# Moving the running sum of two of four experts from VectorE to GpSimd

## The chip, the core and the metric

The kernel runs on one core of a Trainium2 chip. The metric is the device time of one execution in microseconds (us). Three executions of the kernel before took 1468.2, 1460.78 and 1466.7 us; their median is 1466.7 us. Five engines work side by side, each through its own list of instructions in order: PE (TensorE, matmuls), DVE (VectorE), ACT (ScalarE), POOL (GpSimd) and SP (SyncE, which only issues DMAs here). They wait for one another through semaphores.

## What is computed

The reference has three stages; the first works step by step through a sequence of 768 tokens for 4 x 8 heads, the second is a soft mixture of four experts over 3072 tokens, the third sends each token to one of eight experts.

```python
# stage 1, per head
y[t] = q[t] @ state
state = state + beta[t] * outer(k_n[t], v[t] - state.T @ k_n[t])
# stage 2, x of 3072 x 384, four experts, F = 1024
p = domain_probs / (domain_probs.sum(-1, keepdims=True) + 1e-09)
for e in range(4):
    h = np.maximum(x @ w1[e], 0.0)
    out += p[:, e:e + 1] * (h @ w2[e])
# stage 3: token n goes to the expert with the largest logit
out[mask] = gate_w[mask, None] * (np.maximum(x[mask] @ w1[e], 0.0) @ w2[e])
```

The change is in `out += p * (h @ w2)` of stage 2: the sum over the four experts.

## The kernel before

Stage 2 goes through six tiles of 512 tokens, t = 0 to 5. Within a tile, each expert's 1024 hidden columns are cut into eight blocks, so a tile has 4 x 8 = 32 steps s (SPT) and the whole stage 192 steps n (NSTEP). In a step PE does `up(n)` (nine matmuls of 128x512, L1161 to L1163) and then `down(n - 1)` (nine more, L1174 to L1176). Precision is kept by splitting each operand into a high and a low part: ACT makes the high part of the step's weights (`w_high`, L532, tile wsh), and the low part wsl = raw - wsh is made by POOL (`low`, L426) or by DVE (`w_low`, L773). `up(n)` waits for the low part of its own weights, two steps after it was asked for: the loops call `low(n + 2)`. The hidden activations are split the same way by ACT (L536, hh) and DVE (`h_low`, L768, hl).

Stage 1 runs inside stage 2: during tile t the sequence chunk t + 1 is solved, and for chunk t + 2 a 32x32 triangular system is inverted. That inversion (`invert`, L247 and L250) is a chain of 62 dependent instructions of 128x31 up to 128x256 elements. For chunks 2 to 5 it stands on POOL, begun at step 18 + LATE[t] of tiles 0 to 3, with LATE = 3, 1, 0, 0. For the ten steps from there, `low_by_vector` gives the low parts of the weights to DVE, and POOL takes them again afterwards. In tiles 4 and 5 there is no inversion. The order on every engine is written out by the loop over n in `gpsimd`, `vector`, `scalar` and `tensor`; nothing rearranges it.

At the end of an expert, `drain(t, e)` on DVE takes the three PSUM banks ps_yt (128x512 each), multiplies them by the expert's probabilities pb into `acc` (e = 0) or `tmp` (e = 1, 2, 3), L798, and for e = 1, 2, 3 adds tmp to acc, three instructions of 128x512, L805. It stands at the steps s = 8, 16 and 24, and for e = 3 at s = 0 of the next tile. Semaphore dr_ok counts the multiplications; PE waits for it before it overwrites a bank. x2_ok counts the last expert's additions, and sum_ok those of e = 1 and 2.

Of the kernel before, what the change touches and what calls it, by code (L numbers as in the profile page):

```python
# [9 lines left out]
ALU = mybir.AluOpType  # L10
# [14 lines left out]
def f32(ap):  # L25
    return ap.bitcast(F32)


def program(nc, keep, kq_d, kn_d, vn_d, beta_d, probs_d, w_soft, w_top, emb, tau, out, p_d, xs, table):

    NC, _, D, _, _ = kq_d.shape
    E1, NF, _, WCOLS = w_soft.shape
    E2 = w_top.shape[0]
    N, DM = out.shape
    KM = DM // P
# [23 lines left out]
    def sb(stack, name, shape, dt=F32):  # L59
        return stack.enter_context(nc.sbuf_tensor(name, shape, dt))  # L60

    def sem(name):
        return keep.enter_context(nc.semaphore(name))
# [25 lines left out]
    with ExitStack() as soft:  # L89
# [4 lines left out]
        acc = sb(soft, "acc", [P, 2, KM, TOK])  # L94
        tmp = sb(soft, "tmp", [P, KM, TOK])
# [83 lines left out]
    psum_ok, rp_ok, p_set = sem("psum_ok"), sem("rp_ok"), sem("p_set")  # L179
    wh_ok, wlp_ok, wld_ok = sem("wh_ok"), sem("wlp_ok"), sem("wld_ok")  # L180
    s1, hi_ok, lo_ok, s2, y_mm = sem("s1"), sem("hi_ok"), sem("lo_ok"), sem("s2"), sem("y_mm")
    dr_ok, sum_ok, x2_ok = sem("dr_ok"), sem("sum_ok"), sem("x2_ok")
    whT_ok, wlT_ok = sem("whT_ok"), sem("wlT_ok")

    r_const, r_iota, r_dve, r_en, r_enr, r_ent, r_entc = (sem("r_" + n) for n in
# [23 lines left out]
    def att_slot(t, s):  # L209
        return s - LATE[t]  # L210
# [5 lines left out]
    def low_by_vector(n):  # L216
        return n >= 2 and inverting(n - 2)
# [160 lines left out]
    def gpsimd(pool):  # L378
        def constants():
            iota = dict(allow_small_or_imprecise_dtypes=True)  # L380
            nc.gpsimd.memset(upper[:, :], 1.0).then_inc(ones_set, 1)
            nc.gpsimd.memset(upper2[:, :], 1.0).then_inc(ones_set, 1)
            nc.gpsimd.memset(upper3[:, :], 1.0).then_inc(ones_set, 1)
            nc.gpsimd.memset(identR[:, :], 0.0).then_inc(ones_set, 1)
            nc.gpsimd.memset(TT[:, :, :], 0.0).then_inc(zero_set, 1)
            pool.wait_ge(ones_set, 4)
            for mask, base in ((upper, BLK), (upper2, -BLK), (upper3, HALF + BLK)):
                nc.gpsimd.affine_select(out=mask[:, :], in_=mask[:, :], compare_op=ALU.is_gt, fill=0.0, base=base,
                                        pattern=[[1, HALF]], channel_multiplier=-1).then_inc(half_set, 1)
            pool.wait_ge(half_set, 3)  # L390
            nc.gpsimd.affine_select(out=identR[:, :], in_=identR[:, :], compare_op=ALU.not_equal, fill=1.0, base=0,
                                    pattern=[[-1, P]], channel_multiplier=1).then_inc(mask_set, 1)
            pool.wait_ge(mask_set, 1)
            nc.gpsimd.tensor_copy(upper[0:BLK, :], upper2[0:BLK, :]).then_inc(mask_set, 1)
            pool.wait_ge(mask_set, 2)
            nc.gpsimd.tensor_copy(upper[P - BLK:P, :], upper3[P - BLK:P, :]).then_inc(mask_set, 1)
            pool.wait_ge(mask_set, 3)
            nc.gpsimd.memset(ones[:, :], 1.0).then_inc(r_iota, 1)
            nc.gpsimd.memset(after[:, :], 1.0).then_inc(r_iota, 1)
            nc.gpsimd.memset(fill[:, :, :].rearrange("p r c -> p (r c)"), 0.0).then_inc(r_iota, 1)  # L400
            pool.wait_ge(r_iota, 3)
            nc.gpsimd.affine_select(out=after[:, :], in_=after[:, :], compare_op=ALU.is_gt, fill=0.0, base=0,
                                    pattern=[[1, P]], channel_multiplier=-1).then_inc(r_const, 1)
            nc.gpsimd.memset(fill[:, :, 0:1], float(N)).then_inc(r_const, 1)
            nc.gpsimd.memset(zrow[:, :], 0.0).then_inc(r_const, 1)
            nc.gpsimd.iota(rev[:, :], [[-1, E2]], base=E2, channel_multiplier=0, **iota).then_inc(r_const, 1)
            nc.gpsimd.iota(eoff[:, :], [[N, E2]], base=0, channel_multiplier=0, **iota).then_inc(r_const, 1)
            nc.gpsimd.iota(run[:, :], [[N, E2]], base=0, channel_multiplier=0, **iota).then_inc(r_const, 1)
            nc.gpsimd.iota(ids[:, :], [[P, NT], [ROWS, SUB]], base=0, channel_multiplier=1, **iota).then_inc(r_const, 1)
            nc.gpsimd.memset(starts[:, :], 0).then_inc(r_const, 1)  # L410
            nc.gpsimd.memset(oh[:, SUB, :], 0.0).then_inc(r_const, 1)

        def values(c):
            pool.wait_ge(brn_ok, c + 1)
            pool.wait_ge(v_in, 16 * (c + 1))
            nc.gpsimd.tensor_tensor(vN[:, :, :], vN[:, :, :], brn[:, c % 2, :].unsqueeze(2).to_broadcast([P, NU, D]),
                                    ALU.mult).then_inc(v_ok, 1)

        def mask_scores():
            pool.wait_ge(pc_ok, VN)  # L420
            nc.gpsimd.tensor_tensor(PT[:, :, :], PT[:, :, :], upper[:, :].unsqueeze(1).to_broadcast([P, NU, HALF]),
                                    ALU.mult).then_inc(p_ok, VN)

        def low(n):
            pool.wait_ge(wh_ok, n + 1)
            nc.gpsimd.tensor_tensor(wsl[:, n % WB, :], raw[:, n % RB, :], f32(wsh[:, n % WB, :]),  # L426
                                    ALU.subtract).then_inc(wlp_ok, 1)

        def scatter(t):
            pool.wait_ge(r_slot, t + 1)  # L430
            for j in range(SUB):
                nc.gpsimd.indirect_dma_start(  # L432
                    out=table[:, :],
                    out_offset=bass.IndirectOffsetOnAxis(ap=slot_i[:, t % 2, j:j + 1], axis=0),
                    in_=payload[:, t % 2, j, :], in_offset=None).then_inc(scattered[t % 2], 16)

        constants()
        values(0)
        mask_scores()
        for n in range(2):  # L440
            low(n)
        invert(pool, nc.gpsimd, 1)
        values(1)
        for n in range(NSTEP):
            t, s = divmod(n, SPT)
            a = att_slot(t, s)
            if n + 2 < NSTEP and not low_by_vector(n + 2):
                low(n + 2)
            if t >= 1 and s == ROUTE + 9:
                if t == 1:  # L450
                    pool.wait_ge(fill_out, 16)
                scatter(t - 1)
            if a == INV_SLOT and t + 2 < NC:
                values(t + 2)
                invert(pool, nc.gpsimd, t + 2)
        scatter(NT - 1)
        top_gpsimd(pool)

# [187 lines left out]
    def vector(dve):  # L646
# [133 lines left out]
        def drain(t, e):  # L780
            i = E1 * t + e
            dve.wait_ge(pb_in[i % 2], 16 * (i // 2 + 1))
            if e == 0 and t >= 2:
                dve.wait_ge(r_lg, SUB * (t - 1))
            if i == 1:
                dve.wait_ge(fill_out, 16)
                dve.wait_ge(xs_zero, 16)
            if e == 1 and t:
                dve.wait_ge(x2_ok, KM * t)
            if e > 1:  # L790
                dve.wait_ge(sum_ok, KM * ((E1 - 2) * t + e - 1))
            for kk in range(KM):
                if kk < KM - 1:
                    dve.wait_ge(y_mm, (KM - 1) * i + kk + 1)
                else:
                    dve.wait_ge(s2, NF * (i + 1))
                dst = acc[:, t % 2, kk, :] if e == 0 else tmp[:, kk, :]
                nc.vector.tensor_tensor(dst, ps_yt[kk][:, :], pb[:, i % 2, :], ALU.mult).then_inc(dr_ok, 1)  # L798
            for kk in range(KM):
                if e:  # L800
                    dve.wait_ge(dr_ok, KM * i + kk + 1)
                if e > 1:
                    dve.wait_ge(sum_ok, KM * ((E1 - 2) * t + e - 2) + kk + 1)
                if e:
                    nc.vector.tensor_tensor(acc[:, t % 2, kk, :], acc[:, t % 2, kk, :], tmp[:, kk, :],  # L805
                                            ALU.add).then_inc(x2_ok if e == E1 - 1 else sum_ok, 1)

        def probabilities():
            dve.wait_ge(p_in, 16)
# [115 lines left out]
        for n in range(NSTEP):  # L925
            t, s = divmod(n, SPT)
# [569 lines left out]
    @block.gpsimd  # L1496
    def _(pool):
        gpsimd(pool)
# [14 lines left out]
def build(nc, kq, kn, vn, beta, probs, w_soft, w_top, emb, tau, out):  # L1513
    N, DM = out.shape
    xs = nc.dram_tensor("xs_scratch", (N + P, DM), F32, kind="Internal").ap()
    table = nc.dram_tensor("slot_table", (w_top.shape[0] * N, 2), F32, kind="Internal").ap()
    p_d = nc.dram_tensor("p_scratch", tuple(probs.shape), F32, kind="Internal").ap()
    with ExitStack() as keep:  # L1518
        program(nc, keep, kq, kn, vn, beta, probs, w_soft, w_top, emb, tau, out, p_d, xs, table)
# [47 lines left out]
```

## Time and profile before

| | value |
|---|---|
| median of three executions | 1466.7 us |
| profiled execution, its own time | 1468.2 us |
| its span on the core | 1466.4 us |
| PE busy | 1333.3 us, 91% |
| DVE busy | 658.5 us, 45% |
| POOL busy | 592.5 us, 40% |
| ACT busy | 471.2 us, 32% |
| mean granted clock of PE, of full speed | 0.954 |

A row of a group of instructions reads: line, engine, operation, output <- inputs, shapes and count; then busy time and mean duration in ns; then the idle time of that engine just before these instructions, and which engine's instruction ended it. A row in order of time begins with the start in us from the start of the span and the duration in us; neighbours of the same kind are merged (x3), and the idle time ahead of it stands in brackets. A matmul row's duration overlaps the next row's, so PE's speed is read from the distance between starts.

### The profile page before, as it was taken

What the parts mean: (1) busy time and instruction counts of PE and PEld (TensorE: products, weight loads), DVE (VectorE), ACT (ScalarE), POOL (GpSimd) and SP (SyncE); (2) the same over time, 40 slices, a digit from 0 to 9 for tenths busy, and PEclk for the clock granted to TensorE, in tenths of its full rate; (3) what the DMA queues carried; (4) which work ended last, traced back from release to release, by engine and by line L of the source; (5) the groups of instructions that cost most, each with busy time, mean ns of one, the idle gap of its engine ahead of it and who ended that gap; (6) DMA issues with size and microseconds to landing.
All of it is one profiled execution on the core that took longest, in us unless ns stands there. A gap on an engine that the chain in (4) does not pass through costs nothing. (4 is left out here: it accounts for less than half of the span.)

```text
span 1466.4 us, 32026 instructions
## 1 busy us (share of the span) xinstructions
PE 1333.3 (91%) x13279; PEld 1156.3 (79%) x13280; DVE 658.5 (45%) x1084; ACT 471.2 (32%) x794; POOL 592.5 (40%) x624
## 2 busy tenths in 40 slices
PE   4468999899998999999999999999999299999996
PEld 4457888688887888778788788888777299999996
DVE  6833545426453454434545344232652244535342
ACT  2213322253234332243323433334432123424231
POOL 4181337723394235932438423444542222322221
PEclk9589999999999999989999999999998599999998
DMA  8035223533335233262333333335333134334310
GB/s 199 2 106 116 73 79 107 127 113 66 94 112 152 83 60 116 80 159 84 60 101 94 94 91 67 104 104 201 94 104 120 31 118 124 124 131 138 120 30 22
DMA packets 68321, 146.77 MB, mean 100 GB/s; under 512 B 13172, under 2 KB 28977, under 8 KB 67048
## 3 DMA queue, kind: packets, MB, share of 16 engines
q1 hardware_dynamic: 56296, 114.70, 29.0%
q10 hardware_dynamic: 6912, 18.88, 3.8%
q0 software_dynamic: 4992, 11.44, 2.7%
q8 instruction: 94, 1.54, 0.4%
q14 instruction: 27, 0.22, 0.0%
HBM read 132.71 MB, written 11.48 MB: 98 GB/s over the span
## 5 line engine op out<-in xcount | busy, mean ns | idle before, releaser
L426 POOL TENSOR_TENSOR wsl<-raw,wsh 128x768 fp32r<-128x768 f32 x146 | 268.0, 1837 | 511.1 <-ACT wsh L532 505.3
L768 DVE SCALAR_TENSOR_TENSOR hl<-bank,hh 128x512 fp32r<-128x512 f32 x192 | 132.3, 689 | 522.7 <-ACT hh L536 511.5
L536 ACT ACTIVATE hh<-bank 128x512 fp32r<-128x512 f32 x192 | 114.7, 598 | 615.0 <-PE bank L1163 603.2
L1161 PE MATMUL bank<-xhl,wsh 128*128 128x512 f32 x576 | 228.6, 397 | 32.4 <-POOL wsl L426 13.8
L1174 PE MATMUL bank<-hh,wsh 128*128 128x512 f32 x576 | 236.7, 411 | 1.7 <-DVE tmp L798 1.7
L1175 PE MATMUL bank<-hh,wsl 128*128 128x512 f32 x576 | 227.9, 396 | 0.0
L1162 PE MATMUL bank<-xhl,wsh 128*128 128x512 f32 x576 | 227.5, 395 | 0.0
L1176 PE MATMUL bank<-hl,wsh 128*128 128x512 f32 x576 | 227.2, 394 | 0.0
L1163 PE MATMUL bank<-xhl,wsl 128*128 128x512 f32 x576 | 227.0, 394 | 0.0
L532 ACT ACTIVATE wsh<-raw 128x768 fp32r<-128x768 f32 x192 | 160.8, 838 | 13.8 <-DMA raw<-in_w_soft 13.7
L1161 PEld LDWEIGHTS bank<-xhl,wsh 128*128 128x128 f32 x576 | 110.3, 191 | 58.3 <-POOL wsl L426 15.9
L1174 PEld LDWEIGHTS bank<-hh,wsh 128*128 128x128 f32 x576 | 109.9, 191 | 26.6 <-issue 2.1
L1176 PEld LDWEIGHTS bank<-hl,wsh 128*128 128x128 f32 x576 | 109.8, 191 | 24.3
L1163 PEld LDWEIGHTS bank<-xhl,wsl 128*128 128x128 f32 x576 | 110.1, 191 | 23.5
L1162 PEld LDWEIGHTS bank<-xhl,wsh 128*128 128x128 f32 x576 | 110.2, 191 | 23.0
L1175 PEld LDWEIGHTS bank<-hh,wsl 128*128 128x128 f32 x576 | 110.0, 191 | 20.2
L1451 PE MATMUL bank<-gh,wh 128*128 x384 | 109.5, 285 | 3.9 <-DVE gl L1394 2.4
L1453 PE MATMUL bank<-gh,wl 128*128 x384 | 109.1, 284 | 0.0
L1452 PE MATMUL bank<-gl,wh 128*128 x384 | 109.1, 284 | 0.0
L250 POOL TENSOR_TENSOR Tblk<-Tblk,outer 128x31 f32<-128x31 f32 (+15 forms) x155 | 101.8, 657 | 12.2
L1400 DVE SCALAR_TENSOR_TENSOR hl<-bank,hh 128x512 fp32r<-128x512 f32 x64 | 44.1, 690 | 135.7 <-ACT hh L1363 117.5
L247 POOL TENSOR_TENSOR outer<-Lblk,Tblk 128x31 f32<-128x31 f32 (+15 forms) x155 | 88.3, 570 | 34.0 <-DVE Lblk L686 22.3
(205 smaller groups left out, 2127.1 us busy)
## 6 DMA issues: line engine op xcount, KB each, us to landing
raw<-in_w_soft SPq DMA_DIRECT2D x192, 384.0 KB, 3.2
rawT<-in_w_top ACTq DMA_DIRECT2D x48, 384.0 KB, 3.6
kq<-in_kq SPq DMA_DIRECT2D x24, 384.0 KB, 11.7
pb<-p_scratch SPq DMA_DIRECT2D x24, 256.0 KB, 3.8
rawT<-in_w_top SPq DMA_DIRECT2D x16, 384.0 KB, 6.7
kN<-in_kn SPq DMA_DIRECT2D x6, 768.0 KB, 7.0
vN<-in_vn SPq DMA_DIRECT2D x6, 768.0 KB, 5.6
xs_scratch<-xrow SPq DMA_DIRECT2D x20, 192.0 KB, 3.6
```

What stands on the lines that cost most here:

```text
L426: nc.gpsimd.tensor_tensor(wsl[:, n % WB, :], raw[:, n % RB, :], f32(wsh[:, n % WB, :]), ALU.subtract).then_inc(wlp_ok, 1)
L532: nc.scalar.activation(wsh[:, n % WB, :], raw[:, n % RB, :], ACT.Copy).then_inc(wh_ok, 1)
L536: nc.scalar.activation(hh[:, n % 2, :], ps_h[n % 2][:, :], ACT.Relu).then_inc(hi_ok, 1)
L768: nc.vector.scalar_tensor_tensor(out=hl[:, n % 2, :], in0=ps_h[n % 2][:, :], scalar=0.0, in1=f32(hh[:, n % 2, :]), op0=ALU.max, op1=ALU.su ...
L1161: nc.tensor.matmul(o, wsh[:, w, cols], x_hi, start=(kk == 0), stop=False)
L1162: nc.tensor.matmul(o, wsh[:, w, cols], x_lo, start=False, stop=False)
L1163: last = nc.tensor.matmul(o, wsl[:, w, cols], x_hi, start=False, stop=(kk == KM - 1))
L1174: nc.tensor.matmul(o, wsh[:, w, cols], hh[:, n % 2, :], start=(f == 0), stop=False)
L1175: nc.tensor.matmul(o, wsl[:, w, cols], hh[:, n % 2, :], start=False, stop=False)
L1176: last = nc.tensor.matmul(o, wsh[:, w, cols], hl[:, n % 2, :], start=False, stop=(f == NF - 1))
L1451: nc.tensor.matmul(o, wh[par][:, f, rows], x_hi, start=(kk == 0), stop=False)
L1452: nc.tensor.matmul(o, wh[par][:, f, rows], x_lo, start=False, stop=False)
```

## The change

The additions for e = 1 and e = 2 leave DVE. POOL has a new function `add(t, e)`, which waits for the multiplication of each bank (dr_ok) and adds tmp to acc, counted by a new semaphore addp_ok that replaces sum_ok. It is called at s = 16 and s = 24, behind that step's `low(n + 2)`. DVE's multiplications into tmp for e = 2 and e = 3 wait until POOL has taken the previous contents of tmp. The additions for e = 3 stay on DVE.

```diff
+        def add(t, e):
+            for kk in range(KM):
+                pool.wait_ge(dr_ok, KM * (E1 * t + e) + kk + 1)
+                if e == 2:
+                    pool.wait_ge(addp_ok, KM * (2 * t) + kk + 1)
+                nc.gpsimd.tensor_tensor(acc[:, t % 2, kk, :], acc[:, t % 2, kk, :], tmp[:, kk, :],
+                                        ALU.add).then_inc(addp_ok, 1)
...
             if n + 2 < NSTEP and not low_by_vector(n + 2):
                 low(n + 2)
+            if s in (2 * NF, 3 * NF):
+                add(t, s // NF - 1)
...
+            if e >= 2:
+                dve.wait_ge(addp_ok, KM * (2 * t + e - 1))
...
-            if e > 1:
-                dve.wait_ge(sum_ok, KM * ((E1 - 2) * t + e - 1))
...
-            for kk in range(KM):
-                if e:
+            if e == E1 - 1:
+                for kk in range(KM):
                     dve.wait_ge(dr_ok, KM * i + kk + 1)
-                if e > 1:
-                    dve.wait_ge(sum_ok, KM * ((E1 - 2) * t + e - 2) + kk + 1)
-                if e:
                     nc.vector.tensor_tensor(acc[:, t % 2, kk, :], acc[:, t % 2, kk, :], tmp[:, kk, :],
-                                            ALU.add).then_inc(x2_ok if e == E1 - 1 else sum_ok, 1)
+                                            ALU.add).then_inc(x2_ok, 1)
```

On POOL, from the last two instructions of the inversion in tile 0 to the start of the next inversion in tile 1, the list before is this (Tblk and outer belong to the inversion, wsl is the low part of weights, vN and the memset begin the next inversion):

```order
L247 TENSOR_TENSOR outer<-Lblk,Tblk 128x31
L250 TENSOR_TENSOR Tblk<-Tblk,outer 128x31
L426 TENSOR_TENSOR wsl<-raw,wsh 128x768 x14
L432 DMA slot_table<-payload,slot_i 24576x2 x4
L426 TENSOR_TENSOR wsl<-raw,wsh 128x768 x6
L416 TENSOR_TENSOR vN<-vN,brn 128x1536
```

The same stretch of POOL's list with the change:

```order
L247 TENSOR_TENSOR outer<-Lblk,Tblk 128x31
L250 TENSOR_TENSOR Tblk<-Tblk,outer 128x31
L434 TENSOR_TENSOR acc<-acc,tmp 128x512 x3
L426 TENSOR_TENSOR wsl<-raw,wsh 128x768 x14
L440 DMA slot_table<-payload,slot_i 24576x2 x4
L426 TENSOR_TENSOR wsl<-raw,wsh 128x768 x4
L434 TENSOR_TENSOR acc<-acc,tmp 128x512 x3
L426 TENSOR_TENSOR wsl<-raw,wsh 128x768 x2
L416 TENSOR_TENSOR vN<-vN,brn 128x1536
```

Three additions stand directly behind the inversion and ahead of the first low part that POOL makes after it; those are the e = 2 additions of tile 0. The other three, e = 1 of tile 1, stand two low parts ahead of the next inversion. On DVE, around the end of expert 2 inside an inversion (tile 2), the list before has the three multiplications and three additions in a row:

```order
L773 TENSOR_TENSOR wsl<-raw,wsh 128x768
L798 TENSOR_TENSOR tmp<-bank,pb 128x512 x3
L805 TENSOR_TENSOR acc<-acc,tmp 128x512 x3
L768 SCALAR_TENSOR_TENSOR hl<-bank,hh 128x512
L773 TENSOR_TENSOR wsl<-raw,wsh 128x768
```

With the change the same place reads:

```order
L783 TENSOR_TENSOR wsl<-raw,wsh 128x768
L808 TENSOR_TENSOR tmp<-bank,pb 128x512 x3
L778 SCALAR_TENSOR_TENSOR hl<-bank,hh 128x512
L783 TENSOR_TENSOR wsl<-raw,wsh 128x768
```

The three additions are gone from DVE's list there; everything else keeps its place.

## Rows read from the trace of the kernel before

**Rows 1.** Page: busy time, share of the span and instructions of each engine.
```profile
PE 1333.3 (91%) x13279; PEld 1156.3 (79%) x13280; DVE 658.5 (45%) x1084; ACT 471.2 (32%) x794; POOL 592.5 (40%) x624
```
**Rows 2.** Groups by line: busy us, mean ns, idle before and what ended it.
```profile
L1161 PE MATMUL bank<-xhl,wsh 128*128 128x512 f32 x576 | 228.6, 397 | 32.4 <-POOL wsl L426 13.8 <-DMA xhl<-xhl 13.5 <-DVE wsl L773 5.1
L1174 PE MATMUL bank<-hh,wsh 128*128 128x512 f32 x576 | 236.7, 411 | 1.7 <-DVE tmp L798 1.7
L805 DVE TENSOR_TENSOR acc<-acc,tmp 128x512 f32<-128x512 f32 x54 | 39.4, 782 | 0.0
```
**Rows 3.** In order of time, PE: first matmul behind the inversions of tiles 0-3.
```profile
279.46 0.80 PE L1161 MATMUL bank<-xhl,wsh 128*128 128x512 f32 x1 [4.72 <-POOL wsl L426]
...
447.75 0.50 PE L1161 MATMUL bank<-xhl,wsh 128*128 128x512 f32 x1 [2.36 <-POOL wsl L426]
...
622.70 0.50 PE L1161 MATMUL bank<-xhl,wsh 128*128 128x512 f32 x1 [2.88 <-POOL wsl L426]
...
809.40 0.50 PE L1161 MATMUL bank<-xhl,wsh 128*128 128x512 f32 x1 [2.88 <-POOL wsl L426]
```
**Rows 4.** In order of time, POOL: end of the inversion in tile 1.
```profile
445.69 0.25 POOL L250 TENSOR_TENSOR Tblk<-Tblk,outer 128x31 f32<-128x31 f32 x1
445.90 3.59 POOL L426 TENSOR_TENSOR wsl<-raw,wsh 128x768 fp32r<-128x768 f32 x2
```
**Rows 5.** In order of time, POOL: inside tile 1's inversion.
```profile
421.93 0.62 POOL L247 TENSOR_TENSOR outer<-Lblk,Tblk 128x255 f32<-128x255 f32 x1
422.63 0.69 POOL L250 TENSOR_TENSOR Tblk<-Tblk,outer 128x255 f32<-128x255 f32 x1
423.40 0.95 POOL L247 TENSOR_TENSOR outer<-Lblk,Tblk 128x256 f32<-128x256 f32 x1
424.43 1.07 POOL L250 TENSOR_TENSOR Tblk<-Tblk,outer 128x256 f32<-128x256 f32 x1
425.57 0.96 POOL L247 TENSOR_TENSOR outer<-Lblk,Tblk 128x255 f32<-128x255 f32 x1
```
**Rows 6.** In order of time, DVE: tile 1, the end of expert 2.
```profile
423.02 3.02 DVE L805 TENSOR_TENSOR acc<-acc,tmp 128x512 f32<-128x512 f32 x3
```
**Rows 7.** In order of time, POOL: end of the inversion in tile 0.
```profile
275.83 0.72 POOL L247 TENSOR_TENSOR outer<-Lblk,Tblk 128x31 f32<-128x31 f32 x1
276.62 0.58 POOL L250 TENSOR_TENSOR Tblk<-Tblk,outer 128x31 f32<-128x31 f32 x1
277.16 4.02 POOL L426 TENSOR_TENSOR wsl<-raw,wsh 128x768 fp32r<-128x768 f32 x2
```
**Rows 8.** In order of time, DVE: tile 0's last additions.
```profile
275.77 1.98 DVE L805 TENSOR_TENSOR acc<-acc,tmp 128x512 f32<-128x512 f32 x3
```
**Rows 9.** Windows of 6 us: busy us (count) by engine, granted clock, DMA share, GB/s.
```profile
279.40:285.40 6.00, 5.94 (x14) 4.68 (x15) 0.69 (x1) 1.33 (x2) 2.07 (x3) 0.50 0.89 266
...
447.70:453.70 6.00, 5.95 (x26) 4.95 (x27) 0.69 (x1) 1.33 (x2) 3.62 (x2) 1.00 0.44 131
622.60:628.60 6.00, 5.90 (x19) 4.71 (x20) 0.69 (x1) 1.33 (x2) 2.77 (x3) 0.72 0.63 175
809.40:815.40 6.00, 6.00 (x26) 4.96 (x27) 0.69 (x1) 1.33 (x2) 3.59 (x2) 1.00 0.62 175
```
**Rows 10.** Window, same columns: behind the 13.5 us wait at the start.
```profile
97.40:103.40 6.00, 5.95 (x18) 4.79 (x19) 1.14 (x2) 1.33 (x2) 5.22 (x11) 0.67 0.63 194
```
**Rows 11.** In order of time: tile 4 at s = 16, DVE then POOL.
```profile
922.07 1.88 DVE L798 TENSOR_TENSOR tmp<-bank,pb 128x512 f32<-128x512 f32 x3
...
922.24 1.85 POOL L426 TENSOR_TENSOR wsl<-raw,wsh 128x768 fp32r<-128x768 f32 x1 [3.86 <-ACT wsh L532]
926.32 1.83 POOL L426 TENSOR_TENSOR wsl<-raw,wsh 128x768 fp32r<-128x768 f32 x1 [2.23 <-ACT wsh L532]
```
**Rows 12.** In order of time, PE: the `up` that needs the second of these.
```profile
930.83 0.39 PE L1161 MATMUL bank<-xhl,wsh 128*128 128x512 f32 x1
```
**Rows 13.** In order of time: tile 5 at s = 16, PE, DVE and POOL.
```profile
1064.58 0.47 PE L1174 MATMUL bank<-hh,wsh 128*128 128x512 f32 x1 [1.71 <-DVE tmp L798]
...
1063.75 1.87 DVE L798 TENSOR_TENSOR tmp<-bank,pb 128x512 f32<-128x512 f32 x3
...
1064.31 1.85 POOL L426 TENSOR_TENSOR wsl<-raw,wsh 128x768 fp32r<-128x768 f32 x1 [1.30 <-ACT wsh L532]
```
**Rows 14.** In order of time, PE: the `up` behind it in tile 5.
```profile
1070.82 0.39 PE L1161 MATMUL bank<-xhl,wsh 128*128 128x512 f32 x1
```

More of the change, by code:

```diff
@@ L181, in program @@
     s1, hi_ok, lo_ok, s2, y_mm = sem("s1"), sem("hi_ok"), sem("lo_ok"), sem("s2"), sem("y_mm")
-    dr_ok, sum_ok, x2_ok = sem("dr_ok"), sem("sum_ok"), sem("x2_ok")
+    dr_ok, addp_ok, x2_ok = sem("dr_ok"), sem("addp_ok"), sem("x2_ok")
     whT_ok, wlT_ok = sem("whT_ok"), sem("wlT_ok")
```

## The prediction

> **What bounds the kernel now.** I read the shares of the engines first: PE is busy for 91% of the span, DVE for 45%, POOL for 40% [rows 1]. So neither the engine that loses work nor the one that gets it is short of time on average, and moving work between them counts only where PE waits for one of the two. I then read the groups of PE's matmuls with the idle time ahead of them. Behind DVE's multiplications, the start of `drain`, PE loses 1.7 us in the whole run, and no idle time of its matmuls in the 192 steps is ended by an addition (L805). For the low weights of POOL it loses 13.8 us [rows 2]. Last I read that second wait in order of time. 12.8 of the 13.8 us are four waits, of 4.72, 2.36, 2.88 and 2.88 us, one in each of tiles 0 to 3 [rows 3]. Each comes right behind the inversion: in tile 1 POOL's last inversion step starts at 445.69, the first low part follows at 445.90, and PE's `up` starts 1.85 us later, when that part is there [rows 3, 4]. So here POOL, not PE, sets the time, and whatever is put on POOL between the start of the inversion and that low part moves PE one for one.
>
> **What the change adds.** For e = 2 the additions are called at s = 24. In tiles 0 to 3 the inversion has been issued at s = 21, 19, 18 and 18, and it is a chain of 62 instructions that POOL works off first. The additions therefore run behind it and ahead of the low part for which PE already stands still, as the order of POOL's list shows. This is 3 instructions in each of four tiles.
>
> Their duration isn't in the trace: POOL has no 128x512 instruction there. Two like ones bracket it, 0.69 us for 255 elements [rows 5] and 1.80 to 1.83 us for 768 [rows 4, 11]. On the line between them, 0.69 + 257 x (1.83 - 0.69) / 513 = 1.26 us. Three make 3.8 us. Bounds: two thirds of the 768 row gives 1.22 (3.7 for three), the whole 768 row 1.83 (5.5 for three). I take 3.8, since the two rows are the same kind of instruction, at sizes on either side.
>
> **What the change removes.** DVE's three additions in the inversion took 3.02 us [rows 6] where they take 1.98 elsewhere [rows 8], and in the same stretch three inversion steps on POOL took 0.95, 1.07 and 0.96 us where their neighbours of the same size took 0.62 and 0.69 [rows 5]. POOL loses (0.95 - 0.62) + (1.07 - 0.69) + (0.96 - 0.62) = 1.0 us per tile to them, and gets that back. Bounds: 0, if another DVE instruction takes the place, and 2.0, the additions' own time, if POOL were held for all of it. The rows themselves say 1.0.
>
> The Trainium skill, page "SBUF — State Buffer", section "SBUF: two separate sides", says that a DVE instruction with both inputs in SBUF and a GpSimd instruction that reads SBUF exclude each other for a whole instruction. The trace agrees in kind: both sides lose, 1.0 us each. By that rule alone the relief could be the full 2.0 us and the sum below would be 4 us smaller. The page "Perfetto Trace Analysis", section "Optimizing Scalar/DVE Operations", warns that moving work between these two might not help for that reason; it speaks against the change, and I come to the same side from the rows.
>
> So in tiles 1, 2 and 3 the low part comes 3.8 - 1.0 = 2.8 us later, and PE with it. Tile 0 differs. There DVE's e = 3 additions ran from 275.77 on, at the very end of the inversion [rows 8]: the last two steps took 0.72 and 0.58 us instead of about 0.25, and the two low parts 4.02 instead of 3.59 [rows 4, 7], together 1.2 us. Now DVE's multiplications for e = 3 must wait for POOL's additions, so this collision moves behind the low part that counts: 3.8 - 1.0 - 1.2 = 1.6, of which I take 1.5. This new wait is the only one the change adds that holds DVE up. Queued behind it on DVE are the additions for e = 3 and `h_low(33)`. The multiplications start near 279 instead of 274 and all six are done by 283 to 285; `up(33)` cannot start before 281, so `h_low(33)` isn't wanted before 283 and `down(33)` not before 287. PE's `down(32)`, which needs the freed banks, stands behind `up(33)` too. Cost: nothing beyond the 1.5. The direct sum is 1.5 + 3 x 2.8 = 9.9 us.
>
> **The clock.** A wait of PE costs more than its length. After 4.72 us PE was granted 0.50 of full speed, the lower of the levels 1.2 and 2.4 GHz, and did 14 matmuls in 6 us; after the 2.36 us it kept full speed and did 26 [rows 9]. That is 12 matmuls of 6/26 = 0.23 us: 2.8 us lost. After the two waits of 2.88 us it did 19 in one case (1.6 us lost) and 26 in the other. After 13.5 us at the start it did 18, 1.8 us lost [rows 10]. With the change the waits are 6.2, 5.2, 5.7 and 5.7 us. I price a wait of 4.7 us or more at 2.2, the mean of 2.8, 1.8 and a middle value for the phase it happens to fall in; tile 0 already pays it, tile 2 pays 1.6 of it, tiles 1 and 3 nothing. Extra: 0 + 2.2 + 0.6 + 2.2 = 5.0 us. Bounds: 0, and 2.8 + 1.2 + 2.8 = 6.8.
>
> **The other eight places.** At s = 16, in all tiles, and at s = 24 in tiles 4 and 5, POOL isn't in an inversion. In tile 4, the additions start when the low part begun at 922.24 ends, at 924.1, and end at 927.9; the next low part starts then instead of at 926.32 and ends at 929.7, and the `up` that needs it starts at 930.83 [rows 11, 12]. 1.1 us to spare. In the tiles with longer steps there is more. Tile 5 at s = 16 is the tight one: the first multiplication ends at 1064.4, the additions at 1068.2, the low part that began at 1064.31 ends at 1070.05, and with one DVE instruction in the way at 1071.0, against 1070.82 [rows 13, 14]: 0.2 us. The 1.71 us for which PE waits there [rows 13] ends with a multiplication, ahead of the additions, and stays. DVE's own saving, 36 of 54 additions at 0.68 to 0.78 us, some 26 us of busy time, buys nothing, as no PE wait ends with it.
>
> **Sum.** 9.9 + 5.0 + 0.2 = 15.1 us. The profiled execution took 1468.2 us (span 1466.4), so this one would come to 1483.3; it is the slowest of the three, and against their median of 1466.7 the forecast is 1482 us, 1.0% slower.
>
> **Rivals.** Half a per cent, 7.3 us, is about what can be told from no change.
>
> First, the clock adds nothing, because the longer waits fall between its changes, as one of the two of 2.88 us did: 1466.7 + 10.1 = 1477. For it: no fixed price per wait in [rows 9]. Against it: both waits over 4.7 us there had it. Chance 0.17.
>
> Second, the relief is the full 2.0 us in each tile, and the clock adds nothing: 9.9 - 4 = 5.9 us, 1473. This is no change by the bound above. For it: the additions' own length. Against it: POOL's rows lost half of that. Chance 0.09.
>
> Third, faster: POOL's chain in the inversion is held back chiefly by DVE, and freed of it ends early enough that the four waits of 12.8 us go altogether, for 1466.7 - 12.8 = 1454. It decides only from a relief of 3.8 + 2.4 = 6.2 us in a tile, three times what the additions last. Chance 0.02.
>
> Fourth, heavier: the POOL additions cost like the 768 row, 5.5 for three, no relief, full clock price: 1.7 x 4 + 4 + 1.8 more than my sum, 1494. Chance 0.10. My own case has the remaining 0.62.
>
> Range 1472 to 1490. Its lower end is the second rival, its upper end half of the way to the fourth. Faster 0.02, same 0.10 (the second rival and a little of the first), slower 0.88.
>
> **What would show it.** In the profile after: the waits before the first `up` behind the inversions grow to 5 to 6 us in tiles 0 to 3, with POOL's acc additions of about 1.26 us each directly ahead of the two low parts; the inversion steps around s = 24 take 0.6 to 0.7 us; more stretches at half clock follow those waits; no new wait in tiles 4 and 5. It would be wrong if POOL's additions lasted well off 1.26 us, if the inversion ended over 2 us earlier, or if PE waited for DVE's tmp in a tile.

## Result and the profile after

| | before | changed |
|---|---|---|
| median of four timed executions | 1464.6 us | 1483.6 us |
| lowest and highest of them | 1460.8 to 1468.2 | 1478.4 to 1487.1 |
| the profiled execution's own time | 1468.2 us | 1468.2 us |
| its span | 1466.4 us | 1466.5 us |

The changed kernel is slower: ratio 1.0127, 95% interval 1.0085 to 1.017, which is 19 us. The forecast was 1482 us. The two profiled executions, however, took the same time: that of the kernel before is the slowest of its four timed ones, and that of the changed kernel lies 10 us below the fastest of its four. So the comparison of the two spans would have said "no change", and the places have to be compared one by one. First, the page of the changed kernel, its busy shares and its costliest matmuls:

```profile
PE 1333.5 (91%) x13279; PEld 1156.4 (79%) x13280; DVE 640.5 (44%) x1048; ACT 470.8 (32%) x794; POOL 632.9 (43%) x660
...
L1168 PE MATMUL bank<-xhl,wsh 128*128 128x512 f32 x576 | 229.9, 399 | 39.8 <-POOL wsl L426 24.5
L1181 PE MATMUL bank<-hh,wsh 128*128 128x512 f32 x576 | 236.2, 410 | 1.4 <-DVE tmp L808 1.4
```

DVE lost 18 us of busy time and POOL gained 40 [rows 1]. DVE's additions alone fell by 26 us, from 39.4 [rows 2] to 13.2; other DVE instructions took longer, 5.2 us of it the 40 instructions `R<-vN,gks` that the change doesn't touch. The 13.8 us of PE's idle time that ended with POOL's low weights [rows 2] are now 24.5, 10.7 more. Behind DVE's multiplications PE loses 1.4 us, against 1.7 before. (The new lines 1168, 1181, 808 and 812 are 1161, 1174, 798 and 805 of before.)

The groups of DVE and POOL that the change is about, same columns:

```profile
L434 POOL TENSOR_TENSOR acc<-acc,tmp 128x512 f32<-128x512 f32 x36 | 45.8, 1301 | 3.9 <-DVE tmp L808 3.9
L808 DVE TENSOR_TENSOR tmp<-bank,pb 128x512 f32<-128x512 f32 x54 | 34.1, 680 | 6.9 <-POOL acc L434 4.8 <-PE bank L1183 2.0
L812 DVE TENSOR_TENSOR acc<-acc,tmp 128x512 f32<-128x512 f32 x18 | 13.2, 787 | 0.0
```

One addition on POOL takes 1.30 us on average, collisions included. DVE's multiplications now wait 4.8 us for POOL's additions, in tile 0 alone.

PE in order of time, the first matmul behind each inversion, in tiles 0 to 3:

```profile
278.58 0.79 PE L1168 MATMUL bank<-xhl,wsh 128*128 128x512 f32 x1 [5.89 <-POOL wsl L426]
...
448.63 0.80 PE L1168 MATMUL bank<-xhl,wsh 128*128 128x512 f32 x1 [5.88 <-POOL wsl L426]
...
626.30 0.80 PE L1168 MATMUL bank<-xhl,wsh 128*128 128x512 f32 x1 [5.88 <-POOL wsl L426]
...
807.26 0.80 PE L1168 MATMUL bank<-xhl,wsh 128*128 128x512 f32 x1 [5.88 <-POOL wsl L426]
```

These are the four waits of [rows 3], grown from 4.72, 2.36, 2.88 and 2.88 us to 5.9 each. The reason stands in POOL's list at the end of tile 1's inversion:

```profile
442.91 0.25 POOL L250 TENSOR_TENSOR Tblk<-Tblk,outer 128x31 f32<-128x31 f32 x1
443.11 3.70 POOL L434 TENSOR_TENSOR acc<-acc,tmp 128x512 f32<-128x512 f32 x3
446.77 3.59 POOL L426 TENSOR_TENSOR wsl<-raw,wsh 128x768 fp32r<-128x768 f32 x2
```

The low part that used to start when the inversion ended [rows 4] now stands 3.7 us behind it. After each wait PE ran slowly. The windows of 6 us behind the four waits (busy us and count for PE, PEld, DVE, ACT, POOL, then granted clock, DMA share, GB/s):

```profile
278.50:284.50 6.00, 5.92 (x17) 4.71 (x18) 4.25 (x5) 1.33 (x2) 2.08 (x3) 0.62 0.89 268
448.60:454.60 6.00, 5.97 (x16) 4.78 (x17) 0.69 (x1) 1.33 (x2) 2.07 (x2) 0.57 0.47 131
626.30:632.30 6.00, 6.00 (x16) 4.81 (x17) 0.69 (x1) 1.33 (x2) 2.07 (x2) 0.59 0.63 175
807.20:813.20 6.00, 5.94 (x16) 4.73 (x17) 0.69 (x1) 1.33 (x2) 2.07 (x3) 0.59 0.60 175
```

Before, two of the four windows had the full 26 matmuls and clock 1.00 [rows 9]. Now none has: 16 or 17, a mixture of the two levels.

Waits and slow matmuls are read together as the distance between the first `up` matmuls of the steps around the inversions (31 to 34, 62 to 64, 93 to 95 and 125 to 127, 13 steps in all). This sum serves as the yardstick below; I call it the inversion sum. It is 71.6 us in the first profile of before, 72.9 in a second one (e11), 86.8 in the changed kernel and 85.1 in its second profile (e1). The mean rise is 13.7 us.

One place had not been foreseen. In tile 5, step 10, the one-hot instruction that PE's counting waits for took 1.75 us on DVE. It began 0.09 us behind a low part on POOL. DVE, then POOL, then PE:

```profile
1031.27 0.18 DVE L866 TENSOR_REDUCE mk<-key 128x4 f32<-128x32 f32 x1
1031.49 1.75 DVE L867 TENSOR_TENSOR oh<-key,mk 128x32 bf16<-128x32 f32 x1
```

```profile
1031.40 1.80 POOL L426 TENSOR_TENSOR wsl<-raw,wsh 128x768 fp32r<-128x768 f32 x1 [2.24 <-ACT wsh L542]
```

```profile
1033.30 0.19 PE L1211 MATMUL bank<-oh,after 128*128 128x40 bf16 x1 [3.35 <-DVE oh L867]
```

In the first profile of before that instruction starts at 1032.40 and takes 0.19 us, the low part follows it at 1032.50, and PE waits 1.60 us. Here PE waits 3.35 and then runs at a lower clock; the step takes 9.19 us instead of 6.07. Both profiles of the changed kernel have it. Together: 13.7 + 3.1 = 16.8 us, against 19.0 and 17.3 measured.

**Why the two profiled executions agree all the same.** From the first profile of before, the inversion sum rose by 15.2 us and tile 5 by 3.1. The changed kernel's profile gives these 18 us back elsewhere, where the change does nothing: 2.0 us up to step 7, 4.1 in steps 3 and 4 of tiles 2 and 3, 4.6 at step 13 of tiles 1 to 4 (7.7 to 7.9 us before, 6.63 after), 5.2 at step 14 of tile 3 (11.37 before, 6.17 after) and 2.1 behind the last `up`. The first, the second and the last of these differ as much among the thirteen profiles: steps 3 and 4 of tile 2 alone take between 15.6 and 22.5 us. At step 13 PE stands still without waiting for anything recorded. These are two rows of PE in the second profile of before (e11):

```profile
357.50 0.21 PE L1141 MATMUL bank<-PT,U 64*48 64x64 f32 x1 [0.22 <-issue]
...
358.24 0.24 PE L1138 MATMUL bank<-kq,S 48*48 48x64 f32 x1 [0.39 <-issue]
```

Whether the gaps of steps 13 and 14 belong to the program is taken up at e11.

### The profile page after: what moved, and what is told of

Read it like the earlier page. It is cut to its first block and busy times, and to the rows that moved or that the text cites. A ratio compares the mean times of both kernels' runs of the same rounds, so it can differ in the third digit from the quotient of the medians.

```text
span 1466.5 us, 32008 instructions
## 1 busy us (share of the span) xinstructions
PE 1333.5 (91%) x13279; PEld 1156.4 (79%) x13280; DVE 640.5 (44%) x1048; ACT 470.8 (32%) x794; POOL 632.9 (43%) x660
## 5 line engine op out<-in xcount | busy, mean ns | idle before, releaser
L1168 PE MATMUL bank<-xhl,wsh 128*128 128x512 f32 x576 | 229.9, 399 | 39.8 <-POOL wsl L426 24.5
L250 POOL TENSOR_TENSOR Tblk<-Tblk,outer 128x31 f32<-128x31 f32 (+15 forms) x155 | 99.0, 639 | 12.1
## 6 DMA issues: line engine op xcount, KB each, us to landing
kq<-in_kq SPq DMA_DIRECT2D x24, 384.0 KB, 11.3
```

The lines of the kernel that those rows point to most:

```text
L1168: nc.tensor.matmul(o, wsh[:, w, cols], x_hi, start=(kk == 0), stop=False)
```

## Experiments

The theory is that of the prediction: the loss is the second addition (e = 2) standing behind the inversion in tiles 0 to 3, plus the clock behind the waits. The rivals are that the additions cost by themselves, wherever they stand (more POOL work, more contention); that the loss is the new wait of DVE; and that, since the profiled executions agree, it is elsewhere altogether. Each session timed its kernels against runs of before in between. Before's medians of the sessions were 1464.6, 1449.8 (e1 to e4), 1455.4 (e5 to e8) and 1460.6 us (e9 to e11), so the same kernel differs by 1% between sessions. Only ratios within a session are used.

| | ratio, 95% interval | that is, us | inversion sum against 72.3, us |
|---|---|---|---|
| e1, changed kernel again | 1.0119, 1.0096 to 1.0142 | +17.3 | +12.8 |
| e2, only e = 1 on POOL | 0.999, 0.9973 to 1.0007 | -1.4 | +0.3 |
| e3, only e = 2 on POOL | 1.0096, 1.0071 to 1.0121 | +13.9 | +14.3 |
| e4, before with filler | 1.0113, 1.0094 to 1.0133 | +16.4 | +14.6 |
| e5, e = 2 left out in tiles 0 to 3 | 0.9932, 0.9909 to 0.9956 | -9.9 | -4.4 |
| e6, e = 2 behind the low parts | 0.9974, 0.9957 to 0.9992 | -3.8 | -0.8 |
| e7, before, eleven steps | 0.9891, 0.9873 to 0.9908 | -15.9 | -17.5 |
| e8, changed, twelve steps | 0.9917, 0.9901 to 0.9934 | -12.1 | -13.2 |
| e9, POOL adds in tiles 0 to 3 | 1.0084, 1.0061 to 1.0106 | +12.3 | +12.4 |
| e10, before, twelve and eleven | 0.9878, 0.9855 to 0.9901 | -17.8 | -19.1 |
| e11, before again | 0.9998, 0.9976 to 1.0019 | -0.3 | +0.6 |

The third column is the ratio less 1, times before's median in that session. The 72.3 of the fourth is the mean of 71.6 and 72.9. The edits below are shown in part; those of e2, e3, e6, e8 and e9 are set against the changed kernel, those of e4, e5, e7 and e10 against the kernel before.

**e1, the changed kernel unchanged.** No edit.

> The changed kernel once more, for a second profile. The timed runs say +1.3%, yet its profiled execution took 1468.2 us, as that of the kernel before. Theory A: the four waits behind the inversions (5.9 us each) and their stretches at half clock are there in every execution, and the profiled one was quick elsewhere by chance; then this profile shows the same four waits, and the time lies near 1480. Rival B: the waits are usually longer than in that one profile, which fell on a good execution of them; then the waits here differ from 5.9 us.

Measured: +17.3 us, with waits of 5.35, 5.34, 5.37 and 5.37 us. The slowdown repeats. The profile gives 12.8 + 3.1 = 15.9 us of it. The profiled execution took 1466.7 us where some 1480 was expected, but the median of before measured along with it is 1449.8 us. The waits are 0.5 us shorter than in the first profile, so theory A holds with waits that differ between executions.

**e2 and e3, one addition each.** e2 leaves e = 2 on DVE, e3 leaves e = 1 on DVE.

```diff
-            if s in (2 * NF, 3 * NF):
-                add(t, s // NF - 1)
+            if s == 2 * NF:      # e2;  e3: if s == 3 * NF
+                add(t)
```

> Only the additions of e = 1 are on POOL; those of e = 2 stay on DVE. Theory (POOL is late only behind the inversions): no new wait of PE, waits behind the inversions as before (4.7, 2.4, 2.9, 2.9 us), time within 0.2% of before, perhaps +0.2 us from tile 5. Rival (any SBUF work on POOL costs, by collisions with DVE): half of the change's loss, +0.6%.

> Only the additions of e = 2 are on POOL; those of e = 1 stay on DVE. Theory: the whole loss of the change, +1.0 to +1.3%, with four waits of 5.9 us behind the inversions. Rival (both halves share the loss): +0.6%.

Measured: e2 is not told apart from no change; its four waits are 4.72, 2.39, 2.87 and 2.88 us, those of before. e3 has 5.87, 5.40, 5.88 and 5.88 and is 13.9 us slower. The two lines of the pages, e2 first:

```profile
L1169 PE MATMUL bank<-xhl,wsh 128*128 128x512 f32 x576 | 228.5, 397 | 31.8 <-POOL wsl L426 13.8 <-DMA xhl<-xhl 13.7 <-DVE wsl L781 4.2
```

```profile
L1170 PE MATMUL bank<-xhl,wsh 128*128 128x512 f32 x576 | 229.3, 398 | 40.0 <-POOL wsl L426 24.0 <-DMA xhl<-xhl 12.8 <-DVE wsl L782 3.2
```

The 18 additions of e = 1 cost nothing that timing shows, and the 18 of e = 2 cost 13.9 of the 17.3 us of e1: 13.8 against 24.0 us of idle time behind POOL's low weights. The 3.4 us between them are about the loss at step 10 of tile 5, which is absent in e2 and in e3; the intervals of e1 and e3 overlap. "More POOL work as such" falls.

**e4, the same delay without the additions.** The kernel before, with four chained instructions of 256 elements put on POOL behind each of the inversions of tiles 0 to 3; DVE is untouched.

```diff
                 invert(pool, nc.gpsimd, t + 2)
+                pool.wait_ge(inv_step, INV_STEPS * (t + 3))
+                for k in range(4):
+                    nc.gpsimd.tensor_tensor(outer[:, 0:256], outer[:, 0:256], outer[:, 0:256],
+                                            ALU.add).then_inc(filled, 1)
+                    pool.wait_ge(filled, 4 * t + k + 1)
```

> The kernel before with four chained POOL instructions of 128x256 behind each of the inversions of tiles 0 to 3, about 0.77 us each, 3.1 us in all; they compute nothing that is used, and DVE keeps all its additions. Theory (only POOL's time there counts, the moved additions and new semaphores don't): waits of 7.8, 5.5, 6.0 and 6.0 us behind the inversions, +12.4 us for them and some 5 us of half clock, together about +1.2%. Rival (the loss of the change comes from DVE's new wait for tmp or from semaphores): under +0.3%, as nothing of those is in it. Rival for the clock (a longer wait costs only its length): +0.85%.

Measured: +16.4 us with no addition moved and no new wait on DVE. POOL in tile 1:

```profile
442.49 2.68 POOL L459 TENSOR_TENSOR outer<-outer 128x256 f32<-128x256 f32 x4
445.25 3.58 POOL L427 TENSOR_TENSOR wsl<-raw,wsh 128x768 fp32r<-128x768 f32 x2
```

The filler lasted 2.7 us, not the 3.1 expected, and the wait that followed was 5.24 us against 2.36 before. The four waits are 6.84, 5.24, 5.86 and 5.86 us. The rival for the clock, 0.85%, lies below the interval (0.94 to 1.33%): the waits add 11.6 us to the mean of the two profiles of before, the inversion sum 14.6, so 3.0 us are the clock's. A delay at this place is enough for the whole loss; the new wait of DVE isn't needed for it.

**e5, the additions of e = 2 left out.** In tiles 0 to 3 the kernel leaves them out of the sum; neither engine does them.

```diff
             for kk in range(KM):
...
+                if e == 2 and t < 4:
+                    continue
```

> The kernel before without DVE's additions of e = 2 in tiles 0 to 3; these are left out of the sum, nothing takes their place on POOL. It measures the relief alone. In the traces so far the inversion took 43.3 to 43.6 us with these additions and 42.4 to 42.9 without them. Theory (relief of 0.4 to 1.2 us per tile): waits of PE behind the inversions shorter by that each, the half clock behind the first of them gone or less, time 0.2 to 0.5% below before. Rival (full lock, 2 us per tile, as the skill's rule alone would give): waits shorter by 2 us, two or three of them nearly gone, 0.7% or more below before.

Measured: all four waits are 2.2 us, and each inversion lasts 42.88 us, against 44.94, 43.30, 43.55 and 43.55 in tiles 0 to 3 of before. So clearing DVE's additions away gives POOL 0.4 to 0.7 us in tiles 1 to 3. In tile 0 it gives 2.1 us against the first profile of before and 0.7 against the second (43.55 us). The timed gain, 0.68% or 9.9 us, is more than the 0.2 to 0.5% expected and 5.5 us more than the inversion sum shows; that part stays open. By its time the rival of a full lock, 0.7% or more, isn't excluded (the interval is 0.44 to 0.91%); the inversions exclude it in tiles 1 to 3, which are 0.7 us shorter at most and not 2. The half clock behind the first wait is less than in [rows 9], 19 matmuls instead of 14, as the theory had it. The windows behind the first two of the four waits:

```profile
273.40:279.40 6.00, 5.98 (x19) 4.77 (x20) 4.05 (x4) 1.33 (x2) 3.70 (x2) 0.72 0.89 265
438.60:444.60 6.00, 5.97 (x19) 4.85 (x20) 0.69 (x1) 1.33 (x2) 2.35 (x2) 0.72 0.45 131
```

The third window has 26 matmuls at full clock, the fourth 19 again. So waits shorter than the 2.36 us that cost nothing in [rows 9] cost 7 matmuls, 1.6 us, in three places of four.

**e6, the same additions one place later.** In tiles 1 to 3 POOL does them behind the two low parts that PE's next two `up` need, in tiles 4 and 5 at s = 24, and in tile 0 DVE keeps them. The additions of e = 1 stay on DVE.

```diff
+        ADD_STEP = {SPT * t + (3 * NF if t > 3 else INV_SLOT + LATE[t] + 11): t for t in range(1, NT)}
...
-            if s in (2 * NF, 3 * NF):
-                add(t, s // NF - 1)
+            if n in ADD_STEP:
+                add(ADD_STEP[n])
```

> As the kernel that moves only the additions of e = 2, but in tiles 1 to 3 POOL does them behind the first two low parts after the inversion instead of ahead of them; in tile 0 they stay on DVE. Same work on the same engine, another place in its list. Theory (the place is the whole cost): waits of about 4.7, 1.9, 2.3 and 2.3 us, time 0 to 0.4% below before. Rival (POOL's extra work costs wherever it stands): +0.7% or more, as for the kernel with them ahead.

Measured: -3.8 us. POOL in tile 1, then PE behind it:

```profile
440.79 3.60 POOL L426 TENSOR_TENSOR wsl<-raw,wsh 128x768 fp32r<-128x768 f32 x2
444.35 3.78 POOL L433 TENSOR_TENSOR acc<-acc,tmp 128x512 f32<-128x512 f32 x3
448.08 1.85 POOL L426 TENSOR_TENSOR wsl<-raw,wsh 128x768 fp32r<-128x768 f32 x1
```

```profile
442.65 0.50 PE L1175 MATMUL bank<-xhl,wsh 128*128 128x512 f32 x1 [2.22 <-POOL wsl L426]
```

The three additions last 3.78 us, against 3.70 in the changed kernel. But now PE waits 2.22 us instead of 5.88, less than before's 2.36. It is the order of POOL's list that costs, not the work.

**e7 and e8, more low parts for DVE.** While POOL inverts, DVE forms the low parts of ten steps. e7 gives it an eleventh in the kernel before; e8 gives it an eleventh and a twelfth in the changed kernel.

```diff
-        return m < 6 or any(b <= m < b + 10 for b in begun)
+        return m < 6 or any(b <= m < b + 11 for b in begun)    # e8: b + 12
```

> The kernel before, with eleven instead of ten steps of low parts given to DVE in each inversion, so that the first low part for which PE waits is no longer behind the inversion. Theory: the four waits of 12.8 us in all and the half clock behind them (4.4 us) go, -1.1%, perhaps 0.3 us of waiting left in tile 0, where the next low part is wanted 4.1 us later. Rival (another wait is right behind: DVE, the raw weights or the drain): the waits only change their name, under -0.4%.

> The changed kernel with twelve instead of ten steps of low parts given to DVE, so that both the inversion and POOL's additions fit ahead of the low part. Theory: tiles 1 to 3 lose all waiting; in tile 0 the additions of POOL end near 277 while DVE's multiplications of the last expert are wanted from 274, and PE waits some 2.7 us for them (DVE tmp). Against before: -12.8 + 2.7 - 4.4 + 1.8 for a half clock there, -0.9%, about 0.3% above the kernel before with eleven steps. Rival (the freed DVE is worth something once POOL is out of the way): below the kernel before with eleven steps.

Measured: e7 takes 1440.6 us, 1.1% less than before. PE's line and the only wait of over 1 us left behind an inversion, in tile 0, where 0.3 us was expected:

```profile
L1161 PE MATMUL bank<-xhl,wsh 128*128 128x512 f32 x576 | 226.7, 394 | 18.4 <-DMA xhl<-xhl 13.3 <-DVE wsl L773 2.8 <-POOL wsl L426 2.3
```

```profile
279.10 0.50 PE L1161 MATMUL bank<-xhl,wsh 128*128 128x512 f32 x1 [1.28 <-POOL wsl L426]
```

e8 makes the changed kernel 0.8% faster than before, 0.3% above e7 as the theory had it, although all 36 additions stand where they did. What is left of its cost is in tile 0, where PE now waits for DVE's multiplications, which wait for POOL's additions. DVE, then PE:

```profile
278.88 1.89 DVE L808 TENSOR_TENSOR tmp<-bank,pb 128x512 f32<-128x512 f32 x3 [4.93 <-POOL acc L434]
```

```profile
279.71 0.47 PE L1181 MATMUL bank<-hh,wsh 128*128 128x512 f32 x1 [4.14 <-DVE tmp L808]
```

Expected there were 2.7 us. In the changed kernel itself this wait is covered: DVE's multiplications are done at 278.74, 0.2 us after PE's `up` began at 278.58, and `down` stands behind that `up`.

**e9, the additions of tiles 4 and 5 back on DVE.** This tests the part outside the inversions.

```diff
-            if s in (2 * NF, 3 * NF):
+            if s in (2 * NF, 3 * NF) and t < 4:
...
-            if e == E1 - 1:
+            if e == E1 - 1 or e and t >= 4:
```

> The changed kernel with the additions of tiles 4 and 5 left on DVE, so POOL has them only in tiles 0 to 3. Both profiles of the changed kernel show one loss that none of the others has: in tile 5, step 10, a DVE instruction of 0.19 us starts 0.09 us behind a low part on POOL and takes 1.75 us, PE waits 3.35 instead of 1.60 us and runs at half clock. Theory (the loss hangs on a start 0.1 us too late, not on the additions of tiles 4 and 5 as such): their removal gives at most those 3 us, +1.0 to +1.2% against before, with the four waits of 5.4 to 5.9 us unchanged. Rival (the additions of tiles 4 and 5 cost by themselves): +0.8% or less.

Measured: +0.84%, 12.3 us, between the two expectations, and its interval (0.61 to 1.06%) holds both. Step 10 of tile 5 is back at 6.07 us, with waits of 5.37 us at all four inversions and an inversion sum of 84.7, near e1's 85.1. Against the changed kernel's +17.3 and +19 us, some 5 to 7 us are gone, of which step 10 is 3.1; the intervals of the ratios (1.0061 to 1.0106 against 1.0096 to 1.0142) overlap, so timing alone doesn't settle it. e8 speaks against the additions of tiles 4 and 5 as such: it has them where the changed kernel has them, and its step 10 takes 6.07 us.

**e10, a version to beat both.** The kernel before, with twelve steps for DVE in tile 0 and eleven in the others.

```diff
-        return m < 6 or any(b <= m < b + 10 for b in begun)
+        return m < 6 or any(b <= m < b + (11 if t else 12) for t, b in enumerate(begun))
```

> The kernel before with low parts given to DVE for twelve steps in tile 0 and eleven in tiles 1 to 3. With eleven throughout PE still waited 1.3 us in tile 0. Theory: that wait goes too and nothing replaces it, -1.2% against before, the fastest version. Rival (DVE, with one more low part beside the last expert's drain, is late for PE in tile 0): no better than eleven throughout, -1.1% or worse.

Measured: 1440.2 us, 0.9878 of before. PE's line:

```profile
L1161 PE MATMUL bank<-xhl,wsh 128*128 128x512 f32 x576 | 226.5, 393 | 16.2 <-DMA xhl<-xhl 12.2 <-DVE wsl L773 3.1 <-POOL wsl L426 1.0
```

No wait behind an inversion is left. It is faster than both kernels, but can't be told from e7, so its rival isn't excluded.

**e11, the kernel before unchanged.** No edit; it asks whether the gaps of step 13 were chance.

> The kernel before, unchanged, for a second profile. In its first profile tiles 1 to 4 lose 1.1 to 1.2 us each at step 13 and tile 3 another 5.2 us at step 14, in gaps of PE's own issue, which stand in none of the eight other profiles; that is why the first profiles of the two kernels agree in time though the timed runs differ by 1.3%. Theory: those gaps belonged to that execution alone; they are absent here, the waits behind the inversions are 4.7, 2.4, 2.9, 2.9 us again, and the first matmul of the last step is reached 12 us or more earlier than in the first profile. Rival: they belong to this program; then they are here again.

Measured: ratio 0.9998. I had expected that the gaps were an accident of one execution, and that fell: step 13 of tiles 1 to 4 takes 31.0 to 31.1 us in both profiles of before, in e9 and in e10, and 26.5 in each of the other nine. The same four are longer at step 14 of tile 3, by amounts that differ (11.37, 7.21, 9.72 and 8.47 us, against 6.17 in all the others), and in the same four the 40 DVE instructions `R<-vN,gks` take 1.36 us on average, against 1.47 to 1.49.

The gaps needn't go with the program, though. e9, e10 and e11 are three programs, and the whole of one session, which ran on another chip than e1 to e8; e10 has the gaps in tiles 1 to 4 and e7 has none, though the two differ by one low part in tile 0. So they more likely go with the session or its chip. For the first profiles of the two kernels no chip is on record, and the kernel before has the gaps both times and the changed kernel neither time, so the program isn't excluded and the cause stays open. The timed executions fit this. If before had the gaps in every session and e1 to e8 didn't, the timed differences would lie 4.4 us below the inversion sum. They lie on both sides of it: +1.4 in e1 (step 10 of tile 5 taken off), then -1.7, -0.4, +1.8, -5.5, -3.0, +1.6 and +1.1 in e2 to e8, -0.6 on average.

Two other expectations missed. The first wait is 3.42 us here, not 4.7 (the others are 2.37, 2.87 and 2.88), and the first matmul of the last step comes 8.4 us earlier than in the first profile, not 12 or more.

This profile of before also shows how uneven the clock's answer to a short wait is. The window behind the fourth wait, 2.88 us long in both:

```profile
798.40:804.40 6.00, 5.98 (x14) 4.72 (x15) 0.69 (x1) 1.33 (x2) 2.07 (x2) 0.50 0.62 175
```

14 matmuls at half clock, where the first profile had 26 at full clock behind the same wait [rows 9].

## Why the prediction was right

**What bounds it.** Right: PE's waits behind the four inversions decide. e3, e4 and e6 show it from three sides. The additions of e = 2 alone bring the four waits (e3), the same work behind the low parts costs nothing (e6), and a delay without that work costs as much as the change (e4).

**The additions.** Forecast 3.8 us for three, from two neighbouring rows; measured 3.70 in tile 1, 1.26 us each behind all four inversions in both profiles.

**The relief.** Forecast 1.0 us per tile. The inversion of tiles 1 to 3 lasts 42.88 us in the first profile after, 0.4 to 0.7 less than before, and 42.36 in e1, 0.9 to 1.2 less. So 1.0 is inside, at the upper side. Where the rest went can be counted. Set against the shortest that each of the 62 steps takes in eight of the profiles, tile 1's inversion loses 1.0 us beside DVE's three additions before, as forecast, and nothing after. But it also loses time beside nine of DVE's low parts, and this loss goes from 5.6 to 6.0 us in the first profile after, and stays at 5.6 in e1. In tiles 2 and 3 it is 5.8 before, 6.0 and 5.6 after. The error in the reasoning was that the other collisions would stay as they were. Inside tile 1's inversion after, POOL:

```profile
422.26 1.33 POOL L250 TENSOR_TENSOR Tblk<-Tblk,outer 128x256 f32<-128x256 f32 x1
423.66 0.64 POOL L247 TENSOR_TENSOR outer<-Lblk,Tblk 128x255 f32<-128x255 f32 x1
424.38 0.69 POOL L250 TENSOR_TENSOR Tblk<-Tblk,outer 128x255 f32<-128x255 f32 x1
```

Of the three steps that took 0.95 to 1.07 us [rows 5], the first and the third are short now (0.62 and 0.64), and the second takes 1.33 beside a low part of DVE that began at 421.72. The rival of a full 2.0 us relief falls in tiles 1 to 3.

The Trainium skill, page "SBUF — State Buffer", section "SBUF: two separate sides", says that of a DVE instruction with two inputs in SBUF and a GpSimd instruction that reads SBUF, the one that starts first holds the shared ports for its whole length and the other is blocked. The trace agrees in kind: the DVE instruction of 0.19 us that began 0.09 us behind a low part of 1.80 us took 1.75 us. How much comes back when one collision is taken away doesn't follow from it.

**Tile 0.** Forecast +1.5 us, a wait of 6.2. Measured 5.9 and, in e1, 5.35, so +1.2 and +0.6 against the first profile of before; against the 3.42 us of the second they are +2.5 and +1.9. The inversion there is 2.1 to 2.6 us shorter than in the first profile of before and 0.7 to 1.2 than in the second. The e = 3 additions did move away from it, but e5, where they stay, has 42.88 us too: once the inversion ends earlier they start behind it anyway. DVE in tile 0:

```profile
276.85 1.89 DVE L808 TENSOR_TENSOR tmp<-bank,pb 128x512 f32<-128x512 f32 x3 [4.84 <-POOL acc L434]
278.66 3.40 DVE L812 TENSOR_TENSOR acc<-acc,tmp 128x512 f32<-128x512 f32 x3
283.46 0.69 DVE L778 SCALAR_TENSOR_TENSOR hl<-bank,hh 128x512 fp32r<-128x512 f32 x1 [1.40 <-ACT hh L546]
```

DVE's new wait was foreseen, with the multiplications near 279 (they begin at 276.85) and all six done by 283 to 285 (done at 282.1). It costs nothing, as forecast; e8 shows that it is worth 4.1 us of PE's time as soon as the wait in front of it is gone.

**Direct sum.** Forecast 9.9. Against the first profile of before (12.8 us of waits) the four waits add 10.7 us in the first profile after and 8.6 in e1; against the mean of the two profiles of before (12.2) they add 11.3 and 9.2.

**The clock.** Forecast 5.0 us. The inversion sum less the direct sum gives 14.5 - 11.3 = 3.2 and 12.8 - 9.2 = 3.6, both against the mean of the two profiles of before. So this term was taken 1.6 us too high. The price per wait of over 5 us was 8 to 12 matmuls in the eight windows of the two profiles (14 to 18 instead of 26), 1.8 to 2.8 us; 2.2 was a fair mean. The rival "the clock adds nothing" falls. What was taken too low is what before already pays: of the two waits of 2.88 us, the one that went free in the first profile lost 12 matmuls in the second.

**The other eight places.** Right in the places that it named. In tile 4 POOL's additions push the next low part back to 926.70. It ends at 928.5, and the `up` that needs it starts at 929.73 with no wait: 1.2 us to spare, 1.1 forecast. POOL, then PE:

```profile
922.95 3.79 POOL L434 TENSOR_TENSOR acc<-acc,tmp 128x512 f32<-128x512 f32 x3
926.70 1.84 POOL L426 TENSOR_TENSOR wsl<-raw,wsh 128x768 fp32r<-128x768 f32 x1
```

```profile
929.73 0.39 PE L1168 MATMUL bank<-xhl,wsh 128*128 128x512 f32 x1
```

In tile 5 at s = 16 the two steps that follow take 4.17 and 4.21 us instead of 4.10 and 4.08, together 0.2 us, as forecast; the third addition took 2.0 us there. What failed is the claim behind the list, that nothing else is touched: step 10 of tile 5 is none of the eight places, and it lost 3.1 us. The trigger is in the trace: DVE pauses 0.22 us between two small instructions just before, which puts the one-hot instruction behind the low part instead of ahead of it. Why this pause arises in the changed kernel and in e1 and in none of the other eleven profiles isn't settled.

**The sum.** The inversion terms came to 13.7 (10.3 of waits, 3.4 of the clock, means of the two profiles) where 14.9 was forecast, the rest to 3.1 where it was 0.2; the sum is 16.8 against 15.1, and the timed runs say 19.0 and 17.3. So the forecast came near partly by luck: a clock term 1.6 us too high made up for half of the 3.1 us that it didn't have. Two numbers of the prediction don't follow from its own words: 2.8, 1.8 and their middle have the mean 2.3, not 2.2, and half of the way to the fourth rival is 1488, not 1490. Neither matters for the outcome.

**The other rivals.** Faster by the waits going away needed 6.2 us of relief; at most 2.6 was there. The heavy case needed additions of 5.5 us; they last 3.7. The new wait of DVE for tmp, which the prediction priced at nothing, holds up no `down` in tile 0 of the changed kernel, and there is no such wait elsewhere.

## What to carry to other kernels

Before work is moved to an engine that is idle for 60% of the time, look in its list for the instruction that stands ahead of the one the bounding engine waits for: the additions of e = 2 cost 14 us ahead of it and nothing behind it. The remedy for such a wait is in the same rule that made it, here one or two more steps for the other engine (e7, e10), and it was worth as much as the change cost. Two profiled executions that agree prove nothing while a single step differs by 4 us between two executions of one kernel (11.37 and 7.21 us at step 14 of tile 3); compare the places, and let interleaved timings give the sum.

## What the runs showed of the hardware

A DVE instruction of 0.19 us took 1.75 when it began 0.09 us behind a POOL instruction of 1.80, so a shift of 0.2 us in a small instruction became 3.1 us. Waits of PE among matmuls cost clock unevenly, and their length doesn't say how much. A full window of 6 us holds 26 matmuls. Behind the seven waits of 2.2 us (e5; e6 in tiles 1 to 3) the windows held 19 five times and 26 twice, behind those of 2.36 and 2.37 us in before 26 both times, behind before's four of 2.9 us 14 to 19 three times and 26 once, and behind the eight of 5.3 to 5.9 us in the two profiles of the changed kernel never more than 18. Pauses of PE for which no releaser is recorded, 1.1 us at step 13 in each of four tiles, stood in all three profiles of one session and in none of the eight of two others; what they come from is open.
